# A three-layer kernel on one core: batch 1's first spectrum chunk comes second, and the weight splits follow the first tile's reads

## The chip, the core and the metric

The kernel runs on one core of a Trainium2 chip. The core has five engines with an instruction stream each: TensorE (PE: matmuls; PEld: its weight loads), VectorE (DVE), ScalarE (ACT), GpSimd (POOL) and SyncE (SP, which here only issues DMAs). They are synchronised by semaphores. Sixteen DMA engines serve the core. The metric is the device time of one launch in microseconds, the median of several runs.

## The reference

Three layers on x of 2 batches x 3008 positions x 256 channels, all in float32:

```python
X = np.fft.rfft(x, axis=1)                 # layer 1: a filter in the spectrum
y = np.fft.irfft(X * (filt_r + 1j * filt_i)[None], n=3008, axis=1)

x = y.reshape(6016, 256)                   # layer 2: normalised, gated
xn = x / np.sqrt(np.mean(x * x, -1, keepdims=True) + 1e-6) * rms_g
g = xn @ w_gate                            # 256 x 1536
x = (silu(g) * (xn @ w_val)) @ w_out       # 1536 x 256

r = np.maximum(x @ w_in, 0)                # layer 3: 256 x 2048
out = (s * (r * r) + b) @ w_out2           # 2048 x 256
```

The filter is the same for both batches.

## The kernel before, in words

**Spectrum stage.** 3008 = 47 x 64, and the transform is done by tables in four matmul steps. The 256 channels of a batch are cut into 8 chunks, so there are 16 chunks, `q` = 0 to 15, taken in the order of their numbers: first all of batch 0, then all of batch 1. For chunk q: `load_x(q)` brings 384 KB into one of three slots (it waits until step 1 of chunk q-3 has read the slot); TensorE's `step1` (8 matmuls) transforms along 47; ScalarE's `u_out` copies the result out of PSUM; `step2` transforms along 64. VectorE's `products(q, dp)`, dp = 0 and 1, multiplies by the filter with three instructions each; GpSimd's `total(q, dp)` adds the two parts into `spec`; TensorE's `step3(q, dp)` starts the way back and ScalarE's `w_out_copy(q, dp)` puts it into `w_fft` of its batch. `store_w` writes half a batch (four chunks) of that to `by_j` in DRAM, and `load_z` reads it back in another arrangement for `step4`, which finishes the transform for one tile of 376 tokens. There are 16 such tiles.

A filter chunk is 768 KB. There are 8, one for each chunk of a batch. `load_f(n)` loads it, and GpSimd's `sign(n)` then multiplies its imaginary part by signs from the table, before VectorE may use it. Filters stay in SBUF, so that batch 1's chunks (q = 8 to 15) need no load.

TensorE's order in the loop for q from 3: `step2(q)`, `step3(q-1, 0)`, `step1(q+1)` in two halves, `step3(q-1, 1)`. Step 4 of token tiles 0 and 1 is placed into the iterations q = 10, 12, 14 and 15. GpSimd's order is `total(q, 0)`, `total(q, 1)`, then the signing of the filter for a later chunk, or weight splits, or the squares of a token tile.

**Layers 2 and 3.** Each float32 operand is split into a high part (rounded) and a low part (the rest), and `split_product` makes one product of three matmuls. Weights are split on the way: ScalarE makes the high part (`w1_high`, `w1d_high`), and GpSimd (`w1_low`, for the gate and value weights) or VectorE (`w1d_low`, for the down weights) subtracts it from the raw weights. The gate and value weights come in 16 pieces, two for each entry of `ORDER1` = (0, 0), (0, 1), (1, 0), (0, 2), (1, 1), (0, 3), (1, 2), (1, 3), where the first number is 0 for gate and 1 for value and the second is the block of 384 columns. So pieces 0 to 5 hold gate blocks 0 and 1 and value block 0, pieces 6 and 7 gate block 2, pieces 8 and 9 value block 1.

For token tile t and block c of 128 hidden columns (c = 0 to 11), TensorE does `gate_val(t, par, c)`, 12 matmuls, called product c in the prediction, and two blocks later `down(t, par, c)`, 6 matmuls, called down product c. In tile 0, product 0 waits for 6 split pieces, product 3 for 10, product 6 for 14 and product 9 for 16. Between them ScalarE makes the silu, VectorE the product `h` (`hmul`), ScalarE its high part and VectorE its low part (`low`). Down product 0 waits for `low(0, 0)` and for the first down split `w1d_low(0)`. `squares`, `square_sum` and `square_split` on GpSimd prepare the normalisation of a tile, and TensorE's `sums` adds it up.

**What sets the order.** Everything is written out by hand: an engine takes its instructions in the order of the code and stops at the first one whose semaphore isn't there. All DMAs are issued by SyncE, so a DMA behind a waiting one waits too.

Of the kernel before, what the change touches and what calls it, by code (L numbers as in the profile page):

```python
# [21 lines left out]
P = 128  # L22
# [11 lines left out]
PAIRS = 8  # L34
# [12 lines left out]
PIECES1 = 4 * BLOCKS1  # L47
PIECES1D = 2 * BLOCKS1
ORDER1 = ((0, 0), (0, 1), (1, 0), (0, 2), (1, 1), (0, 3), (1, 2), (1, 3))
PIECE2O = 512  # L50
# [46 lines left out]
def build(nc, by_j, x, filt, tab, small, w_gate, w_val, w_out, w_in2, w_out2, out):  # L97
    with ExitStack() as ctx:
# [139 lines left out]
        def _(sp):  # L238
# [6 lines left out]
            def load_f(n):  # L245
                sp.dma_start(f_tiles[n][:].rearrange("p k c -> p (k c)"), filt[n]).then_inc(f_in[n], 16)

            def store_w(b, half):

                sp.wait_ge(w_done, CHUNKS * (2 * b + half + 1))  # L250
                sp.dma_start(by_j[b, half].rearrange("p j d -> p (j d)"),
                             w_fft[b][:, half].rearrange("p j d -> p (j d)")).then_inc(w_stored[b][half], 16)
# [11 lines left out]
            sp.dma_start(tabs[:, 0:TB2], tab[:, 0:TB2]).then_inc(tab1_in, 16)  # L264
            load_x(1)
            load_f(0)
            sp.dma_start(tabs[:, TB2:], tab[:, TB2:]).then_inc(tab2_in, 16)
            load_x(2)
            load_f(1)
            load_f(2)  # L270
            for q in range(3, 8):
                load_x(q)
                load_f(q)
            load_x(8)
            load_x(9)
            store_w(0, 0)
            load_x(10)
            sp.dma_start(consts[:], small).then_inc(consts_in, 16)
            load_x(11)
            sp.wait_ge(w_stored[0][0], 16)  # L280
            for t in range(2):
                load_z(0, 0, t * GROUPS * XROWS, t)
            load_gate(0)
            store_w(0, 1)
            load_x(12)
            load_x(13)
# [244 lines left out]
        def _(a):  # L531
# [7 lines left out]
            def w_out_copy(q, dp):  # L539
                b, n = q // CHUNKS, q % CHUNKS  # L540
                a.wait_ge(s3_mm, 2 * q + dp + 1)
                n, d0 = n * HALVES // CHUNKS, (2 * n + dp) * PAIRS * HALVES % P
                nc.scalar.copy(w_fft[b][:, n, :, d0:d0 + PAIRS * HALVES],
                               bank[6][:, 0:COLS].rearrange("p (d j) -> p j d", j=NJ)).then_inc(w_done, 1)
# [206 lines left out]
        def _(dve):  # L751
            nc.vector.memset(warm[:], 1.0).then_inc(warm_set, 1)
            def products(q, dp):

                dve.wait_ge(s2_mm, q + 1)
                if q < CHUNKS:
                    dve.wait_ge(f_signed, q + 1)
                if q:
                    dve.wait_ge(spec_done, 2 * (q - 1) + dp + 1)
                xs = bank[2 + 2 * (q % 2) + dp]  # L760
                f = f_tiles[q % CHUNKS]
                cols = slice(dp * COLS, (dp + 1) * COLS)
# [57 lines left out]
            hmul(0, 0)  # L820
            hmul(0, 1)
            low(0, 0)
            w1d_low(0)

# [74 lines left out]
        def _(gp):  # L899
# [44 lines left out]
            gp.wait_ge(tab1_in, 16)  # L944
            for n in range(2):
                sign(n)
            for q in range(ALL):
                total(q, 0)
                total(q, 1)
                if q + 2 < CHUNKS:  # L950
                    sign(q + 2)
                elif q == 11:
                    for i in range(3):
                        w1_low(i)
                elif q == 12:
                    squares(0)
                    square_sum(0)
                    square_split(0)
                elif q == 13:
                    for i in range(3, 6):  # L960
                        w1_low(i)
                elif q == 15:
                    w1_low(6)
                    w1_low(7)

            def body(t, par, last):
# [4 lines left out]
                if is0(t):  # L971
                    for i in range(8, PIECES1):
                        w1_low(i)
                    gp.wait_ge(in2_in, 16)
# [53 lines left out]
```

## Time and profile before

| | us |
|---|---|
| median of 3 runs (lowest, highest) | 1257.45 (1256.34, 1257.88) |
| profiled execution, its own time | 1262.11 |
| its span, first to last instruction | 1260.3 |
| TensorE busy in it | 1245.2 |
| VectorE, ScalarE, GpSimd busy | 679.3, 554.1, 161.9 |

The spectrum stage takes about the first 100 us, layers 2 and 3 the rest. The mean granted TensorE clock is 0.995 of full speed. A timeline row gives start, duration, engine, line, operation, output and inputs, and how often; in brackets stands for how long the engine was idle before it and what released it. Rows of neighbouring instructions of a kind are merged. The trace counts a float32 matmul of the spectrum stage twice, so that one step 2 of a chunk, 4 matmuls, is a row of x8. "Old time axis" below means the times of this profiled execution.

### The profile page before, as it was taken

How to read it: one execution, taken by the hardware profiler on the slowest of the kernel's cores; microseconds unless marked ns; L12 is line 12 of the kernel's file. 1: busy time of each engine (PE TensorE's matmuls, PEld its weight loads, DVE VectorE, ACT ScalarE, POOL GpSimd, SP SyncE). 2: the span in 40 equal slices, each digit the busy share in tenths (PEclk: the TensorE clock that was granted, in tenths of full speed). 3: DMA queues.
4: the chain of work that ended last, by engine and by line, in shares of the span. 5: the costliest groups of instructions: out<-in, count | busy, mean ns of one | idle time of the engine just before them, and what ended most of it. 6: DMA issues, size and time to landing. Idle time of an engine off the chain costs nothing.

```text
span 1260.3 us, 20452 instructions
## 1 busy us (share of the span) xinstructions
PE 1245.2 (99%) x7268; PEld 1214.0 (96%) x7268; DVE 679.3 (54%) x1141; ACT 554.1 (44%) x1111; POOL 161.9 (13%) x167
## 2 busy tenths in 40 slices
PE   8998999999999999999999999999999999999998
PEld 5677999999999999999999999999999999999998
DVE  4675455444454444544454375555555555555555
ACT  2365333333434334343344364555454545554554
POOL 5665111011110111101120030000000000000000
PEclk9998999999999999999999999999999999999999
DMA  9863000000000000000010000000000000000000
GB/s 236 272 217 154 14 13 14 1 13 12 13 12 1 11 12 12 12 3 10 0 67 1 1 1 14 13 13 12 12 12 12 12 12 12 12 12 12 13 6 20
DMA packets 22519, 41.07 MB, mean 33 GB/s; under 512 B 1872, under 2 KB 18384, under 8 KB 21456
## 3 DMA queue, kind: packets, MB, share of 16 engines
q1 hardware_dynamic: 22480, 40.55, 10.4%
q8 instruction: 24, 0.39, 0.1%
q14 instruction: 15, 0.12, 0.0%
HBM read 28.10 MB, written 12.45 MB: 32 GB/s over the span
## 4 chain that ended last, share of the span: by engine, by line
PE 91%; POOL 4%; issue 3%; DMA 1%; SPq 0%; DVE 0%; POOLq 0%
PE bank L388 30%; PE bank L389 30%; PE bank L390 30%; POOL spec L916 2%; PE bank L373 2%; DMA f<-filt 1%; POOL gate_lo L921 0%; POOL val_lo L921 0%; POOL sq L931 0%; PE bank L385 0%; PE bank L384 0%; POOL f L909 0%; POOL sq L935 0%; SPq L243 0%; POOL ss_lo L942 0%
## 5 line engine op out<-in xcount | busy, mean ns | idle before, releaser
L801 DVE TENSOR_TENSOR h<-bank,act 128x376 f32<-128x376 f32 x192 | 104.5, 545 | 314.8 <-PE bank L390 307.7
L832 DVE SCALAR_TENSOR_TENSOR h<-act,consts 128x376 f32<-128x376 f32 x256 | 159.6, 623 | 189.5 <-ACT act L667 185.5
L573 ACT ACTIVATE act<-bank 128x376 f32<-128x376 f32 x192 | 92.9, 484 | 363.3 <-PE bank L390 363.0
L667 ACT ACTIVATE act<-bank 128x376 f32<-128x376 f32 x256 | 124.0, 484 | 224.0 <-PE bank L390 223.9
L390 PE MATMUL bank<-h_hi,out_lo 128*128 128x376 f32 x512 | 171.4, 335 | 0.0
L389 PE MATMUL bank<-h_lo,out_hi 128*128 128x376 f32 x512 | 171.4, 335 | 0.0
L388 PE MATMUL bank<-xn_hi,in_hi 128*128 128x376 f32 x512 | 171.2, 334 | 0.2 <-issue 0.2
L388 PE MATMUL bank<-h_hi,out_hi 128*128 128x376 f32 x512 | 171.2, 334 | 0.0
L389 PE MATMUL bank<-xn_lo,in_hi 128*128 128x376 f32 x512 | 171.1, 334 | 0.0
L390 PE MATMUL bank<-xn_hi,in_lo 128*128 128x376 f32 x512 | 170.3, 333 | 0.0
L838 DVE SCALAR_TENSOR_TENSOR h_lo<-h,consts,h_hi 128x376 fp32r<-128x376 f32 x256 | 157.7, 616 | 0.2 <-ACT h_hi L676 0.2
L676 ACT ACTIVATE h_hi<-h,consts 128x376 fp32r<-128x376 f32 x256 | 154.2, 603 | 1.9 <-DVE h L832 1.9
L388 PE MATMUL bank<-xn_hi,gate_hi 128*128 128x376 f32 x384 | 131.6, 343 | 2.8 <-POOL val_lo L921 2.7
L388 PE MATMUL bank<-h_hi,down_hi 128*128 128x376 f32 x384 | 128.7, 335 | 1.7 <-DVE down_lo L775 1.7
L389 PE MATMUL bank<-xn_lo,val_hi 128*128 128x376 f32 x384 | 129.3, 337 | 0.0
L390 PE MATMUL bank<-h_hi,down_lo 128*128 128x376 f32 x384 | 128.9, 336 | 0.0
L389 PE MATMUL bank<-h_lo,down_hi 128*128 128x376 f32 x384 | 128.8, 335 | 0.0
L388 PE MATMUL bank<-xn_hi,val_hi 128*128 128x376 f32 x384 | 128.7, 335 | 0.0
L389 PE MATMUL bank<-xn_lo,gate_hi 128*128 128x376 f32 x384 | 128.6, 335 | 0.0
L390 PE MATMUL bank<-xn_hi,val_lo 128*128 128x376 f32 x384 | 128.6, 335 | 0.0
L390 PE MATMUL bank<-xn_hi,gate_lo 128*128 128x376 f32 x384 | 128.5, 335 | 0.0
L809 DVE TENSOR_TENSOR h_lo<-h,h_hi 128x376 fp32r<-128x376 f32 x192 | 118.4, 617 | 1.4 <-ACT h_hi L582 1.3
(79 smaller groups left out, 2041.3 us busy)
## 6 DMA issues: line engine op xcount, KB each, us to landing
x_ring<-x SPq DMA_DIRECT2D x16, 384.0 KB, 7.5
f<-filt SPq DMA_DIRECT2D x8, 768.0 KB, 15.0
by_j<-w_b SPq DMA_DIRECT2D x4, 1536.0 KB, 6.1
z_ring<-by_j SPq DMA_DIRECT2D x32, 192.0 KB, 2.8
out<-staged SPq DMA_DIRECT2D x32, 188.0 KB, 1.9
in_raw<-w_in SPq DMA_DIRECT2D x1, 2048.0 KB, 8.7
out_raw<-w_out SPq DMA_DIRECT2D x1, 2048.0 KB, 7.7
gate_raw<-w_gate SPq DMA_DIRECT2D x2, 768.0 KB, 7.2
```

What stands on the lines that cost most here:

```text
L373: mm = nc.tensor.matmul(bank[7][:, k * BM:(k + 1) * BM], z_ring[:, par, half, k], s4m, start=True, stop=True)
L388: nc.tensor.matmul(acc, hi, xh, start=first, stop=False)
L389: nc.tensor.matmul(acc, hi, xl, start=False, stop=False)
L390: return nc.tensor.matmul(acc, lo, xh, start=False, stop=final)
L573: nc.scalar.activation(act[:, c % 2], bank[2 * (c % 2)][:, 0:TILE], ACT.Silu).then_inc(silu_done, 1)
L667: nc.scalar.activation(act[:, c % 2], bank[c % 4][:, 0:TILE], ACT.Relu).then_inc(relu_done, 1)
L676: nc.scalar.activation(h_hi[:, c % 4], h[:, c % 2], ACT.Identity, bias=bi2).then_inc(gh_done, 1)
L801: nc.vector.tensor_tensor(h[:, c % 2], bank[2 * (c % 2) + 1][:, 0:TILE], act[:, c % 2], ALU.mult).then_inc(hmul_done, 1)
L809: nc.vector.tensor_tensor(h_lo[:, c % 4], h[:, c % 2], h_hi[:, c % 4].bitcast(F32), ALU.subtract).then_inc(hl_done, 1)
L832: nc.vector.scalar_tensor_tensor(out=h[:, c % 2], in0=act[:, c % 2], scalar=sc2, in1=act[:, c % 2], op0=ALU.mult, op1=ALU.mult).then_inc(q ...
L838: nc.vector.scalar_tensor_tensor(out=h_lo[:, c % 4], in0=h[:, c % 2], scalar=bi2, in1=h_hi[:, c % 4].bitcast(F32), op0=ALU.add, op1=ALU.su ...
L916: nc.gpsimd.tensor_tensor(spec[:, q % 2, dp], prod[:, dp, 0], prod[:, dp, 1], ALU.add).then_inc(spec_done, 1)
```

## The change

1. The 16 chunks are taken in the order `ORDER`: batch 0 chunk 0, batch 1 chunk 0, then batch 0 chunks 1 to 7, then batch 1 chunks 1 to 7. `q` now counts places in this order. Place 0 and place 1 both use filter 0, and place q up to 8 uses filter q-1. The host arranges x in that order. `products`, `w_out_copy` and `store_w` look up their chunk in `ORDER`; so the stores of batch 0's halves wait for 10 and 18 copies, where 8 and 16 were waited for.
2. SyncE issues the second table before filter 0, and filter q-1 behind x chunk q. `load_x(12)` stands ahead of the first wait for a store.
3. GpSimd signs one filter before its loop, and then filter q+1 behind the sums of chunk q.
4. GpSimd's splits of the gate and value weights stand in other places: two pieces after chunk 11 (three before), four after chunk 13 (three), two after chunk 14 (none), two after chunk 15 (two, but now pieces 8 and 9).
5. VectorE does `w1d_low(0)` before `low(0, 0)`.

```diff
+ORDER = [(0, 0), (1, 0)] + [(0, n) for n in range(1, CHUNKS)] + [(1, n) for n in range(1, CHUNKS)]
...
-                sp.wait_ge(w_done, CHUNKS * (2 * b + half + 1))
+                sp.wait_ge(w_done, 2 * ORDER.index((b, CHUNKS // HALVES * (half + 1) - 1)) + 2)
...
             load_x(1)
+            sp.dma_start(tabs[:, TB2:], tab[:, TB2:]).then_inc(tab2_in, 16)
             load_f(0)
-            sp.dma_start(tabs[:, TB2:], tab[:, TB2:]).then_inc(tab2_in, 16)
-            load_x(2)
-            load_f(1)
-            load_f(2)
-            for q in range(3, 8):
+            for q in range(2, 9):
                 load_x(q)
-                load_f(q)
-            load_x(8)
+                load_f(q - 1)
             load_x(9)
             store_w(0, 0)
             load_x(10)
             sp.dma_start(consts[:], small).then_inc(consts_in, 16)
             load_x(11)
+            load_x(12)
             sp.wait_ge(w_stored[0][0], 16)
...
             store_w(0, 1)
-            load_x(12)
             load_x(13)
...
             def w_out_copy(q, dp):
-                b, n = q // CHUNKS, q % CHUNKS
+                b, n = ORDER[q]
...
             def products(q, dp):
                 dve.wait_ge(s2_mm, q + 1)
-                if q < CHUNKS:
-                    dve.wait_ge(f_signed, q + 1)
+                dve.wait_ge(f_signed, ORDER[q][1] + 1)
...
-                f = f_tiles[q % CHUNKS]
+                f = f_tiles[ORDER[q][1]]
...
             hmul(0, 1)
+            w1d_low(0)
             low(0, 0)
-            w1d_low(0)
...
-            for n in range(2):
-                sign(n)
+            sign(0)
             for q in range(ALL):
                 total(q, 0)
                 total(q, 1)
-                if q + 2 < CHUNKS:
-                    sign(q + 2)
+                if q + 1 < CHUNKS:
+                    sign(q + 1)
                 elif q == 11:
-                    for i in range(3):
+                    for i in range(2):
                         w1_low(i)
...
                 elif q == 13:
-                    for i in range(3, 6):
+                    for i in range(2, 6):
                         w1_low(i)
-                elif q == 15:
-                    w1_low(6)
-                    w1_low(7)
+                elif q >= 14:
+                    w1_low(2 * (q - 11))
+                    w1_low(2 * (q - 11) + 1)
...
-                    for i in range(8, PIECES1):
+                    for i in range(10, PIECES1):
                         w1_low(i)
```

On SyncE at the program's start (`f_50` is filter 0, `f_51` filter 1 and so on; `tabs` of 128x384 is the second table), before:

```order
L243 DMA x_ring<-x 96x1024
L264 DMA tabs<-tab 128x120
L243 DMA x_ring<-x 96x1024
L246 DMA f_50<-filt 128x1536
L267 DMA tabs<-tab 128x384
L243 DMA x_ring<-x 96x1024
L246 DMA f_51<-filt 128x1536
L246 DMA f_52<-filt 128x1536
L243 DMA x_ring<-x 96x1024
L246 DMA f_53<-filt 128x1536
```

and now:

```order
L244 DMA x_ring<-x 96x1024
L265 DMA tabs<-tab 128x120
L244 DMA x_ring<-x 96x1024
L267 DMA tabs<-tab 128x384
L247 DMA f_50<-filt 128x1536
L244 DMA x_ring<-x 96x1024
L247 DMA f_51<-filt 128x1536
L244 DMA x_ring<-x 96x1024
L247 DMA f_52<-filt 128x1536
L244 DMA x_ring<-x 96x1024
L247 DMA f_53<-filt 128x1536
```

The second table has moved ahead of filter 0, and there is an x chunk between any two filters.

On GpSimd from the sums of chunk 13 (`spec`) to the splits behind the squares of token tile 1 (`sq`, `ss_hi`, `ss_lo`), before:

```order
L916 TENSOR_TENSOR spec<-prod 128x384 x2
L921 TENSOR_TENSOR gate_lo<-gate_raw,gate_hi 128x384
L921 TENSOR_TENSOR val_lo<-val_raw,val_hi 128x384 x2
L916 TENSOR_TENSOR spec<-prod 128x384 x4
L921 TENSOR_TENSOR gate_lo<-gate_raw,gate_hi 128x384 x2
L931 TENSOR_TENSOR sq<-y 128x752
L935 TENSOR_TENSOR sq<-sq 128x376
L940 CAST ss_hi<-sq 128x376
L942 TENSOR_TENSOR ss_lo<-sq,ss_hi 128x376
L921 TENSOR_TENSOR val_lo<-val_raw,val_hi 128x384 x2
```

and now:

```order
L912 TENSOR_TENSOR spec<-prod 128x384 x2
L917 TENSOR_TENSOR gate_lo<-gate_raw,gate_hi 128x384 x2
L917 TENSOR_TENSOR val_lo<-val_raw,val_hi 128x384 x2
L912 TENSOR_TENSOR spec<-prod 128x384 x2
L917 TENSOR_TENSOR gate_lo<-gate_raw,gate_hi 128x384 x2
L912 TENSOR_TENSOR spec<-prod 128x384 x2
L917 TENSOR_TENSOR val_lo<-val_raw,val_hi 128x384 x2
L927 TENSOR_TENSOR sq<-y 128x752
L931 TENSOR_TENSOR sq<-sq 128x376
L936 CAST ss_hi<-sq 128x376
L938 TENSOR_TENSOR ss_lo<-sq,ss_hi 128x376
```

Pieces 6 and 7 (`gate_lo`) have moved between the sums of chunks 14 and 15, and pieces 8 and 9 (`val_lo`) from behind the squares of tile 1 to ahead of them.

On VectorE right behind the last products, with the first blocks of token tile 0, before:

```order
L801 TENSOR_TENSOR h<-bank,act 128x376 x2
L809 TENSOR_TENSOR h_lo<-h,h_hi 128x376
L775 TENSOR_TENSOR down_lo<-down_raw,down_hi 128x384
L801 TENSOR_TENSOR h<-bank,act 128x376
L809 TENSOR_TENSOR h_lo<-h,h_hi 128x376
L775 TENSOR_TENSOR down_lo<-down_raw,down_hi 128x384
```

and now:

```order
L797 TENSOR_TENSOR h<-bank,act 128x376 x2
L771 TENSOR_TENSOR down_lo<-down_raw,down_hi 128x384
L805 TENSOR_TENSOR h_lo<-h,h_hi 128x376
L797 TENSOR_TENSOR h<-bank,act 128x376
L805 TENSOR_TENSOR h_lo<-h,h_hi 128x376
L771 TENSOR_TENSOR down_lo<-down_raw,down_hi 128x384
```

The first down split and the low part of the first h have changed places.

## Rows read from the trace of the kernel before

**Rows 1.** Of the page, part 1: busy time, share of span, instructions.

```profile
PE 1245.2 (99%) x7268; PEld 1214.0 (96%) x7268; DVE 679.3 (54%) x1141; ACT 554.1 (44%) x1111; POOL 161.9 (13%) x167
```

**Rows 2.** View of waits, TensorE, whole span: us in total, times, longest.

```profile
PE bank L388 <- POOL val_lo L921: 2.7, 1, 2.7
...
PE bank L362 <- POOL spec L916: 2.4, 4, 0.9
PE bank L388 <- DVE down_lo L775: 1.7, 1, 1.7
```

**Rows 3.** Windows: busy us of each engine, granted clock, DMA share, GB/s.

```profile
20.00:45.00 25.00, 23.51 (x139) 15.41 (x136) 17.27 (x32) 9.09 (x19) 18.12 (x15) 1.00 1.02 240
13.40:16.30 2.90, 2.90 (x12) 1.28 (x8) 2.02 (x4) 0.00 (x0) 1.01 (x1) 0.50 1.08 338
105.60:112.20 6.60, 6.11 (x19) 6.11 (x20) 1.89 (x3) 2.11 (x5) 4.41 (x5) 0.50 0.78 268
```

**Rows 4.** Timeline, GpSimd, start: start us, us, instruction, idle before and releaser.

```profile
10.96 1.80 POOL L909 TENSOR_TENSOR f<-f,tabs 128x768 f32<-128x768 f32 x1 [6.95 <-DMA f<-filt]
...
21.31 1.95 POOL L916 TENSOR_TENSOR spec<-prod 128x384 f32<-128x384 f32 x2
...
45.37 1.81 POOL L909 TENSOR_TENSOR f<-f,tabs 128x768 f32<-128x768 f32 x1 [2.11 <-DMA f<-filt]
```

**Rows 5.** Timeline, TensorE, spectrum stage.

```profile
12.22 4.48 PE L352 MATMUL bank<-u_ring,tabs 64*128 64x384 f32 x16 [2.47 <-DMA tabs<-tab]
...
23.11 1.92 PE L341 MATMUL bank<-tabs,x_ring 128*128 128x96 f32 x16
...
25.63 1.56 PE L352 MATMUL bank<-u_ring,tabs 64*128 64x384 f32 x8
...
51.46 1.56 PE L352 MATMUL bank<-u_ring,tabs 64*128 64x384 f32 x8
...
56.22 1.56 PE L352 MATMUL bank<-u_ring,tabs 64*128 64x384 f32 x8
...
72.90 1.13 PE L373 MATMUL bank<-consts,z_ring 96*128 96x94 f32 x8
```

**Rows 6.** Timeline, VectorE, first and last product of chunk 0.

```profile
14.19 0.56 DVE L763 TENSOR_TENSOR prod<-bank,f 128x384 f32<-128x384 f32 x1 [12.78 <-PE bank L352]
...
17.13 0.55 DVE L765 TENSOR_TENSOR prod<-bank,f 64x384 f32<-64x384 f32 x1
```

**Rows 7.** Timeline, SyncE's queue, batch 0's second store and its z loads.

```profile
56.84 0.37 SPq L251 DMA_DIRECT2D by_j<-w_b  x1
...
63.12 0.85 SPq L255 DMA_DIRECT2D z_ring<-by_j  x2
```

**Rows 8.** Of the page, part 6: count, KB each, us from issue to landing.

```profile
z_ring<-by_j SPq DMA_DIRECT2D x32, 192.0 KB, 2.8
```

**Rows 9.** Timeline, GpSimd, first token tile.

```profile
97.16 2.00 POOL L921 TENSOR_TENSOR gate_lo<-gate_raw,gate_hi 128x384 fp32r<-128x384 f32 x2
...
104.10 1.93 POOL L921 TENSOR_TENSOR val_lo<-val_raw,val_hi 128x384 fp32r<-128x384 f32 x2
```

**Rows 10.** Timeline, VectorE, first token tile.

```profile
98.47 1.09 DVE L809 TENSOR_TENSOR h_lo<-h,h_hi 128x376 fp32r<-128x376 f32 x1 [1.30 <-ACT h_hi L582]
99.49 1.79 DVE L775 TENSOR_TENSOR down_lo<-down_raw,down_hi 128x384 fp32r<-128x384 f32 x1
```

**Rows 11.** Timeline, TensorE, first token tile.

```profile
101.42 0.41 PE L388 MATMUL bank<-h_hi,down_hi 128*128 128x376 f32 x1 [1.68 <-DVE down_lo L775]
101.67 0.34 PE L389 MATMUL bank<-h_lo,down_hi 128*128 128x376 f32 x1
...
102.53 0.81 PE L362 MATMUL bank<-spec,tabs 128*128 128x384 f32 x2
106.09 0.68 PE L388 MATMUL bank<-xn_hi,gate_hi 128*128 128x376 f32 x1 [2.75 <-POOL val_lo L921]
...
111.90 0.51 PE L388 MATMUL bank<-xn_hi,gate_hi 128*128 128x376 f32 x1
```

## What the change was predicted to do

> **What bounds the kernel now.** I read the page first. It gives TensorE as busy for 99% of the span [rows 1], so the only things that can change the time are the stretches in which TensorE waits and those in which it works at the lower of its two clock levels. The view of waits then says where TensorE stands still: 2.7 us once for the GpSimd split of the value weights, 2.4 us over four waits for the GpSimd sum of the spectrum, 1.7 us once for the VectorE split of the down weights [rows 2]. With the 2.47 us of wait for the second table [rows 5] nearly all lies before 110 us; the remaining 1,150 us is matmul behind matmul, which the change doesn't touch. So I read the first 112 us only, by windows and by timeline, engine by engine.
>
> The windows show two things [rows 3]. From 20 to 45 us the DMA engines are busy for their whole time (share 1.02, 240 GB/s): the spectrum stage is paced by transfers there. And there are two stretches at granted clock 0.50, which is 1.2 GHz, from about 13.4 to 16.3 us and from 105.6 to 112.2 us. Each came with or right after an idle gap of TensorE, of 2.47 us and of 2.75 us with 1.68 us shortly before it [rows 5, 11].
>
> GpSimd shows how the transfers pace the stage [rows 4]: it waits for filter n to land, signs it in 1.8 us, and only then makes the sum that lets the chunk before go on. The last filter lands at 45.37 us. TensorE's iteration 3 (counted by the chunk of its step 2) starts at 25.63 us and iteration 8 at 51.46 us; from 8 to 9 it takes 4.76 us, with TensorE without a gap [rows 5]. Five iterations at that pace are 23.8 us, and they took 25.83 us: about 2.0 us is lost to filters there, and the rest of the loss lies ahead of iteration 3.
>
> **Part 1, one filter fewer in front of every chunk.** Chunk q now needs filter q-1. Ahead of chunk q's filter stand 768 KB less, which at the 240 GB/s of the window is 3.3 us. That is the ceiling of this part if transfers alone decide. What decides first is the start, so I walk it.
>
> The second table now follows the second x chunk and has no filter in front. It must land by about 9.7 us, where TensorE ends step 1 of both chunks (12.22 less 2.47 idle). Only 192 KB, under 1 us, come after an x chunk that has been used by then, so I take this wait of 2.47 us as gone. Filter 0 takes the place that the table had: the same bytes have passed, so I let it land when the table did, at 12.22 us [rows 5]; it may be 0.4 us earlier, since filter 0 alone came at 10.96 us and only 192 KB are added. From there: sign 1.80 us [rows 4], to 14.02. The six products of chunk 0 take 3.49 us (14.19 to 17.68, [rows 6]), to 17.54. The second sum is 0.98 us (half of a pair of 1.95 to 1.96), to 18.5. Then GpSimd signs filter 1 (1.8 us; it has landed by then, since no byte more stands in front of it than before, and chunk 1's sum, which comes after its signing and three products of 1.7 us, began at 21.31, so that it lay there by 17.8), to 20.3, and makes the first sum of chunk 1, to 21.3. Before, that sum ended at 22.29 us (start 21.31), and iteration 3 began 3.34 us later. So iteration 3 now starts at about 24.65 us, 1.0 us earlier.
>
> Iterations 3 to 7 then need filters 2 to 6 in the place of 3 to 7, and TensorE's own pace of 4.76 us puts iteration 8 at 48.45 us, 3.0 us earlier. Filter 7 is the check: the bytes up to it are those of before plus one x chunk (384 KB, 1.6 us), so it lands at about 47.0 us; sign, sum and hand-over (2.8 us) give 49.8 us, and step 3 that needs it comes 1.5 us into iteration 8, at 49.95. That is hardly a margin. I take **2.8 us** for this part, with 1.8 us (filter 7 a microsecond late) and 3.3 us (the bytes' ceiling) as its ends.
>
> From iteration 8 on, what comes earlier must not run into loads that don't. The store of batch 0's second half waits for a chunk later than before (18 copies for 16): issued at 56.84 us before, now 4.76 us later by place and 2.8 us earlier by pace, 58.8 us. The z loads behind it could go 6.3 us after the store (56.84 to 63.12, [rows 7]), so now at 65.1, and land 2.8 us after their issue [rows 8], by 68.3 with the second issue. TensorE's step 4 for them stood at 72.90 us [rows 5] and stands at 70.1 now. Clear by 1.8 us. The x chunk that moved ahead of the first z loads, and the gate weights behind those, have more room by the same working, so these edits cost 0.
>
> **Part 2, weight splits in the order of reading.** TensorE's gate and value product number 3 waits for pieces 8 and 9. GpSimd made them at 104.10 us, behind the squares and sums of token tile 1, which nobody needed then [rows 9]. It now makes pieces 6 and 7 ahead of chunk 15's sums and 8 and 9 behind them. Pieces 6 and 7 ended at 99.16 (97.16 plus 2.00); the same work in another order ends there at the latest, and since the timeline has GpSimd idle between the sums of chunks 14 and 15 for most of the two pieces' time, I take 97.6. Pieces 8 and 9 are then done at about 99.6 us on the old time axis, 101.1 at the latest. TensorE comes to product 3 at 102.1 (1.92 us after down product 0 starts, as 103.34 stands to 101.42, [rows 11]; part 3 has that start). ScalarE has their high halves by then: it makes them ahead of the second silu, whose product VectorE had finished at 97.17 us (98.47 less 1.30 idle, [rows 10]). Chunk 15's sums are over by 97.6, and their first matmul stood at 98.9 (101.42 less 1.68 idle less its own 0.8). So the wait of 2.75 us goes. What is queued behind, the squares, takes its 5 us (99.16 to 104.10) from 99.6 and is done at 104.7; TensorE's sums of tile 1 come after product 5, at about 111.
>
> **Part 3, the two VectorE instructions exchanged.** Before, VectorE stood idle for 1.30 us for the high part of h, then made the low part (1.09 us), then the down split (1.79 us), and TensorE's down product began at 101.42 us after 1.68 us of waiting [rows 10, 11]. Now the split runs in that idle time: 97.17 plus 1.79 is 98.96, plus 1.09 is 100.05, and TensorE starts at about 100.15. The wait shrinks to 0.4 us. Its ends: 1.68 (the exchange brings nothing) and 0 (the split is fast). Both instructions read two operands in SBUF, and they took 1.79 us beside a busy GpSimd. The Trainium skill, in "GPSIMD Engine Reference", Key points, says that GpSimd shares its SBUF interfaces with VectorE, with contention for instructions of two SBUF inputs. The trace fits it with the 1.79 us, and the rule speaks against any hope of a fast split here, since the change puts more GpSimd work ahead of 97 us and not less.
>
> **Part 4, the clock.** With 4.43 us of idle time shrunk to 0.4, the second low stretch has no gap in front of it. Products 3 with their down product, 18 matmuls from 106.09 to 111.90 us, took 5.81 us [rows 11]; five matmuls between 101.67 and 102.53 us stood 0.172 us apart, so 18 take 3.10. That is 2.7 us, and 0.2 us for the three matmuls after 111.90 that ran partly slow. Parts 2 to 4 together: 2.75 + 1.68 - 0.4 + 2.9 = **6.9 us**; ends 5.6 (the exchange brings nothing) and 7.3.
>
> Sum: 2.8 + 6.9 = 9.7 us. The profiled execution took 1262.1 us, so it would take 1252.4; the median of the runs shown is 4.7 us lower, and I take the same difference off it: 1257.45 - 9.7 = **1247.8 us**. Its own range, with the ends of both terms, is 1246.8 to 1250.1.
>
> **Rivals.** First, **the clock falls at the start again.** The change removes one gap but makes two: TensorE ends step 2 of two chunks at 12.9 us (9.75 and twice 1.56), has 1.9 us of step 1 for chunk 2 [rows 5], and stands until chunk 0's first sum at about 17 (half the products and 0.98 us after 14.02), 2.2 us in all; then it waits about 1.5 us more, to 21.3, for the sum behind the signing. Before, 2.47 us in one piece was enough [rows 3, 5]. Against it: work lies between these pieces. A low stretch of 3 us there doubles about 1.5 us of work: gain 8.2 us, 1249.3. At the length of the second one (6.6 us) it costs 3.3: 1251.1. A sentence apart: the Trainium skill, "TensorE: Matmul & The Clock Gate", Part 1, says that how many matmuls run slow at a kernel's start varies from run to run; by that rule this rival would come in some runs and not in others.
>
> Second, **the start's gain doesn't last**: filter 7, or a transfer further back, is late by as much as the loop gained, and TensorE meets chunk 15 no earlier. For it speaks that the margins above are 0.1 to 1.8 us; against it, that the bytes are fewer. Gain 6.9, 1250.6 us.
>
> Third, **the split wait comes back one step later.** Product 6 needs pieces 12 and 13, which GpSimd now makes after squares and pieces 10 and 11, at about 108.7 us, and TensorE arrives at 111.7. A GpSimd slowed by VectorE could lose those 3 us and more. Gain 4 to 5.6 us in all, 1252.6.
>
> Fourth, **slower**: the z loads. SP issues in order, and step 4 of tile 0 is in TensorE's fixed order. If the store, now a chunk later, and the loads queued behind it slip by more than 1.8 us, TensorE waits in iteration 12, each us costs one, the clock may fall on top (3 us), and everything behind on SP (x chunks, value weights) slips too. It decides the sign from a slip of 1.8 + 9.7 - 3 = 8.5 us; at 12 us the time is about 1261. The DMA engines were far from full there, so I give it little.
>
> **Chances.** Forecast 0.62, clock at the start 0.15, start's gain lost 0.08, split wait returns 0.06, no change for a reason that I don't see 0.05, slower 0.04. 0.2% is 2.5 us, about what a measurement can tell; all of the first four are past it, so faster 0.91, same 0.05, slower 0.04. The range goes up to 1252.0, which takes in the first three cases and part of the fourth, and down to 1245.8: both terms at their high ends (10.6 us) are 1246.8, and a microsecond for the spread of the runs.
>
> **What would show it.** The wait for the second table gone and filter 0 landing near 12.2 us; iteration 3 near 24.7 and iteration 8 near 48.5 us, with no longer wait there than 0.3 us; step 4 of tile 0 without a wait; the value split ending near 97 us on the new axis; down product 0 waiting under 0.6 us, product 3 not at all, and a granted clock of 1.00 from the start's end on. I am wrong if a clock of 0.50 shows between 17 and 30 us, if iteration 8 starts after 49.7, or if a new wait on GpSimd stands at product 6.

## The result, and the profile after

| | before | after |
|---|---|---|
| median of 4 runs each (lowest, highest), us | 1257.66 (1256.34, 1259.76) | 1249.22 (1248.59, 1250.03) |
| profiled execution, its own time | 1262.11 | 1250.03 |
| its span | 1260.3 | 1248.2 |

The ratio is 0.9932, with a 95% interval of 0.9914 to 0.9949: 8.6 us faster (6.4 to 10.8), and 1249.2 us measured against 1247.8 forecast. The two profiled executions differ by 12.1 us and the medians by 8.4; where the rest comes from turned out to be the interesting part.

Of the page after, part 1, which answers to [rows 1]:

```profile
PE 1239.7 (99%) x7268; PEld 1210.3 (97%) x7268; DVE 680.4 (55%) x1141; ACT 554.1 (44%) x1111; POOL 164.1 (13%) x167
```

TensorE's waits in the kernel after, over the whole span (us in total, times, longest), which answer to [rows 2]:

```profile
PE bank L359 <- POOL spec L912: 2.6, 2, 1.4
PE bank L330 <- DVE warm L749: 1.5, 1, 1.5
PE bank L381 <- POOL ss_lo L938: 0.6, 1, 0.6
PE bank L338 <- DMA x_ring<-x: 0.3, 1, 0.3
```

The waits for the value split, the down split and the second table are gone. The 1.5 us for `warm` lie at the program's very start, before the first matmul, and were the same in the kernel before. What is left otherwise of more than 0.6 us is the wait for GpSimd's sum, twice, before the first `step3` of chunks 0 and 1: the two gaps that the prediction's first rival had.

Windows of the kernel after (busy time of each engine, granted clock, DMA share, GB/s). The first holds the first of those gaps, the others answer to [rows 3]:

```profile
12.00:16.00 4.00, 2.51 (x18) 2.16 (x18) 3.18 (x6) 0.96 (x2) 1.55 (x2) 1.00 1.04 257
20.00:45.00 25.00, 25.00 (x147) 16.67 (x147) 17.70 (x32) 9.78 (x21) 20.94 (x17) 1.00 1.02 277
95.00:112.00 17.00, 17.00 (x97) 16.50 (x96) 13.63 (x16) 11.50 (x23) 12.94 (x13) 1.00 0.57 217
```

The clock is 1.00 in all of them. From 20 to 45 us TensorE is busy for all of its time, and the DMA engines still are too, at 277 GB/s where the profiled execution of before had 240.

TensorE's timeline after (start, duration, instruction, in brackets the idle time before it), with the rows that answer to [rows 5, 11]. In order they are step 2 of the first two chunks in one row, the first step 3 of chunks 0 and 1, iterations 3 and 8, step 4 of tile 0, down product 0, and products 3 and 4:

```profile
8.95 2.85 PE L349 MATMUL bank<-u_ring,tabs 64*128 64x384 f32 x16
...
15.52 0.91 PE L359 MATMUL bank<-spec,tabs 128*128 128x384 f32 x2 [1.40 <-POOL spec L912]
...
20.00 0.91 PE L359 MATMUL bank<-spec,tabs 128*128 128x384 f32 x2 [1.24 <-POOL spec L912]
...
23.28 1.56 PE L349 MATMUL bank<-u_ring,tabs 64*128 64x384 f32 x8
...
47.10 1.56 PE L349 MATMUL bank<-u_ring,tabs 64*128 64x384 f32 x8
...
68.55 1.13 PE L370 MATMUL bank<-consts,z_ring 96*128 96x94 f32 x8
...
94.82 0.59 PE L385 MATMUL bank<-h_hi,down_hi 128*128 128x376 f32 x1
...
96.46 0.62 PE L385 MATMUL bank<-xn_hi,gate_hi 128*128 128x376 f32 x1
...
99.97 0.34 PE L385 MATMUL bank<-xn_hi,gate_hi 128*128 128x376 f32 x1
```

Iteration 8 starts at 47.10 us instead of 51.46. Down product 0 and product 3 follow without any gap, and product 4, which began at 111.90 us, begins at 99.97.

GpSimd and VectorE after, which answer to [rows 4, 9, 10]: filter 0 and filter 1 signed; the splits of pieces 6 and 7 and of 8 and 9; the down split ahead of the low part of h:

```profile
10.75 1.81 POOL L905 TENSOR_TENSOR f<-f,tabs 128x768 f32<-128x768 f32 x1 [6.74 <-DMA f<-filt]
...
17.19 1.81 POOL L905 TENSOR_TENSOR f<-f,tabs 128x768 f32<-128x768 f32 x1
...
89.15 1.98 POOL L917 TENSOR_TENSOR gate_lo<-gate_raw,gate_hi 128x384 fp32r<-128x384 f32 x2
...
93.02 2.60 POOL L917 TENSOR_TENSOR val_lo<-val_raw,val_hi 128x384 fp32r<-128x384 f32 x2
95.59 1.43 POOL L927 TENSOR_TENSOR sq<-y 128x752 f32<-128x752 f32 x1
```

```profile
92.58 0.90 DVE L771 TENSOR_TENSOR down_lo<-down_raw,down_hi 128x384 fp32r<-128x384 f32 x1
94.13 0.63 DVE L805 TENSOR_TENSOR h_lo<-h,h_hi 128x376 fp32r<-128x376 f32 x1 [0.65 <-ACT h_hi L579]
```

Pieces 8 and 9 are done at 95.62 us, 0.8 us before product 3 would read them, and the squares of tile 1 start behind them.

### The profile page after: what moved, and what is told of

It reads as the page before. It is cut to its first block, busy times and chain, and to the rows that moved or that the text cites. A ratio compares the mean times of both kernels' runs of the same rounds, so it can differ in the third digit from the quotient of the medians.

```text
span 1248.2 us, 20452 instructions
## 1 busy us (share of the span) xinstructions
PE 1239.7 (99%) x7268; PEld 1210.3 (97%) x7268; DVE 680.4 (55%) x1141; ACT 554.1 (44%) x1111; POOL 164.1 (13%) x167
## 4 chain that ended last, share of the span: by engine, by line
PE 95%; POOL 2%; issue 1%; DMA 1%; DVE 1%; SPq 0%; POOLq 0%; DVEq 0%
PE bank L385 30%; PE bank L386 30%; PE bank L387 30%; PE bank L370 2%; POOL spec L912 1%; PE bank L359 1%; PE bank L349 1%; PE bank L338 1%; DMA f<-filt 1%; POOL f L905 0%; PE bank L381 0%; PE bank L382 0%; DVE prod L761 0%; DVE prod L760 0%; POOL gate_lo L917 0%
```

## The experiments

All were timed in turns with the kernel before on the same chip. In each, "us under before" is the ratio applied to 1256.5 us.

**The kernel before once more.**

> The kernel before once more, with its own profile. Theory A (the clock theory): the profiled execution of before (1262.1 us) was 4.6 us over the median of its runs because its two stretches at granted clock 0.50 aren't the same in every execution; then the executions here spread over some 3 to 6 us, the mean granted clock goes with the time (a longer execution shows a lower clock), and this profile shows low stretches of another length or place. Rival B: a profiled execution is simply 4.6 us longer; then this one takes about 1262 again with the same two low stretches, and all others 1257 to 1258 at one clock.

Measured: 1256.53 us in 12 runs and 1256.53 in 29 of the kernel before beside them (ratio 0.9997, 0.9986 to 1.0007). The profiled execution took 1256.44 us with a mean clock of 1.000. TensorE's waits and timeline in it:

```profile
PE bank L388 <- POOL val_lo L921: 2.8, 1, 2.8
PE bank L362 <- POOL spec L916: 1.8, 1, 1.8
PE bank L352 <- DMA tabs<-tab: 1.7, 1, 1.7
PE bank L388 <- DVE down_lo L775: 1.7, 1, 1.7
```

```profile
17.54 0.91 PE L362 MATMUL bank<-spec,tabs 128*128 128x384 f32 x2 [1.81 <-POOL spec L916]
...
24.69 1.56 PE L352 MATMUL bank<-u_ring,tabs 64*128 64x384 f32 x8
...
48.52 1.56 PE L352 MATMUL bank<-u_ring,tabs 64*128 64x384 f32 x8
...
103.17 0.44 PE L388 MATMUL bank<-xn_hi,gate_hi 128*128 128x376 f32 x1 [2.75 <-POOL val_lo L921]
...
106.39 0.34 PE L388 MATMUL bank<-xn_hi,gate_hi 128*128 128x376 f32 x1
```

The two waits in front of the first tile's products stand to a tenth of a microsecond as in [rows 2], but the clock never falls: products 3 and their down product take 3.22 us (103.17 to 106.39) where they took 5.81 in [rows 11]. And the stage isn't paced by filters: from iteration 3 to 8 it takes 23.83 us, which is TensorE's own pace, against 25.83 in [rows 5]. So theory A holds, and more than it said: the one trace on which my sum rested was the slow end in two ways. Over all 73 executions of the kernel before in these experiments, 22 have a mean granted clock of 1.000, with a median of 1255.2 us, and 51 have 0.999 or less, with 1257.1. None of the 73 took as long as the profiled 1262.11.

**The chunk order alone.**

```diff
 (of the kernel after)
-            w1d_low(0)
             low(0, 0)
+            w1d_low(0)
...
-                    for i in range(2):
+                    for i in range(3):
                         w1_low(i)
...
```

The second edit, with three more of its kind behind it, puts GpSimd's splits back where the kernel before has them.

> Only the new order of chunks, filters, tables and signs; GpSimd's splits and VectorE's two instructions as before. Traces of before and after say that iteration 8 starts 4.4 us earlier (51.46 to 47.10), so by theory A the time falls by 4.4 us less what of the start's low clock an average execution didn't have: 3 to 4.4 us, and the waits for the value split (2.7 us) and the down split (1.7 us) stand as before. Rival B: by my prediction's sum it is 2.8 us. A third, that the parts aren't additive: the end loses what the start gains, under 1.5 us.

Measured: 1255.16 us, ratio 0.9982 (0.9973 to 0.9992): 2.3 us under before (1.0 to 3.4). TensorE's waits and iterations 3 and 8:

```profile
PE bank L385 <- POOL val_lo L917: 2.7, 1, 2.7
...
PE bank L385 <- DVE down_lo L771: 1.7, 1, 1.7
```

```profile
22.07 1.56 PE L349 MATMUL bank<-u_ring,tabs 64*128 64x384 f32 x8
...
45.89 1.56 PE L349 MATMUL bank<-u_ring,tabs 64*128 64x384 f32 x8
```

Both end waits are where they were, and in this trace the clock did fall behind them (0.50 from 102 to 104 us). The interval holds the prediction's 2.8 us, and theory A's 3 to 4.4 only at its edge.

**The splits and the exchange alone.**

```diff
 (of the kernel before)
+            w1d_low(0)
             low(0, 0)
-            w1d_low(0)
...
-                elif q == 15:
-                    w1_low(6)
-                    w1_low(7)
+                elif q >= 14:
+                    w1_low(2 * (q - 11))
+                    w1_low(2 * (q - 11) + 1)
...
```

The numbers of pieces after chunks 11 and 13 are those of the change too (two and four), and tile 1's loop begins with piece 10.

> Only GpSimd's splits at their new places and VectorE's exchange, chunks in the old order. Both waits in token tile 0 should be gone: 4.4 us, and where an execution had the low clock behind them up to 2.9 us more. Theory A, with low clock in only part of the executions of before: 4.4 to 6 us in the median, and a profile with granted clock 1.00 from 20 us on. Rival B (low stretch in every execution of before): 6.9 to 7.7 us.

Measured: 1250.03 us, ratio 0.9943 (0.9927 to 0.9958), 7.2 us under before (5.3 to 9.2). A second time, beside the changed kernel on one chip:

> Splits and exchange alone, chunks in the old order, beside the changed kernel. Theory A: 1 to 1.5 us over the changed kernel. Rival B: the same time, so the last 2.3 us that the chunk order won alone (with the old splits) came from somewhere that the new splits win too, such as the clock.

> The changed kernel, on one chip with the splits and exchange alone. Theory A, the chunk order brings 1.5 us more on top of them (from the traces: iteration 8 starts 36.4 us after filter 0 lands in the new order, 37.9 or more in the old, and filter 0 lands up to 0.8 us later): about 1 to 1.5 us under the other. Rival B, nothing on top: within 0.5 us of it.

Measured: 1250.60 us, ratio 0.9954 (0.9940 to 0.9968), 5.8 us under before (4.0 to 7.5), and the changed kernel 1249.06 us, ratio 0.9942 (0.9928 to 0.9955). For the splits and the exchange the first timing lies with rival B (6.9 to 7.7) and the second with theory A (4.4 to 6); each interval reaches into both, so these times alone don't decide between them.

The chunk order on top brings 1.5 us here, as theory A had it. Each of the five runs of the changed kernel is under each of the other's five, while the ratios' intervals overlap; with all runs of the two kernels together the difference is 1.2 (1250.53 in 11 runs, 1249.29 in 14). So the size is less sure than the sign. The second trace of the splits alone shows something else that the chunk order changes. Filter 0 lands at 9.27 us in it, and TensorE's timeline has:

```profile
16.30 1.49 PE L362 MATMUL bank<-spec,tabs 128*128 128x384 f32 x2 [1.43 <-POOL spec L916]
17.73 2.62 PE L352 MATMUL bank<-u_ring,tabs 64*128 64x384 f32 x8
...
48.92 1.56 PE L352 MATMUL bank<-u_ring,tabs 64*128 64x384 f32 x8
```

The clock falls behind the gap at chunk 0's step 3 (the window from 16 to 18 us has 0.63), and iteration 8 starts 39.65 us after filter 0 landed. In the first trace of this kernel the clock stays at 1.00 and it is 37.92 (8.30 to 46.22 us).

**The changed kernel beside others.**

> The changed kernel once more, beside the others. The two parts measured alone were 2.3 us (chunk order) and 7.2 us (splits and exchange). Theory A, the parts add up: 9.4 us under before, with every mean granted clock at 1.0 because no gap in front of the first token tile is left. Rival B, the parts overlap: what the chunk order wins in an average execution is mostly gone once the splits are in place; then about 8 us or less, as the first timing said (8.4).

Measured: 1249.51 us, ratio 0.9941 (0.9929 to 0.9954), 7.4 us under before (5.8 to 8.9). 2.3 plus 7.2 is 9.5, over the interval, while with the second timing of the splits (5.8 us) the parts add to 8.1. I can't tell from these whether they overlap. In 13 of the changed kernel's 14 executions the mean clock is 1.000 (the other, the profiled one here with 0.999, has no low stretch before 1240 us); in the kernel before it was so in 22 of 73.

**The gaps filled, the waits left.**

```diff
+            def fill(n):
+                for _ in range(n):
+                    nc.tensor.matmul(bank[7][:, 0:TILE], ones_r[:], xn_hi[:, 0, 0], start=True, stop=True)
...
+                    if is0(t) and c == 1:
+                        pe.wait_ge(y_done, 4)
+                        fill(14)
...
+                        fill(8)
                     down(t, par, c)
```

The 8 stand ahead of down product 0, the 14 ahead of product 3, both in tile 0 alone.

> The kernel before with 8 extra matmuls in front of down product 0 and 14 in front of product 3 of token tile 0, whose results aren't used; they fill the two waits (1.4 of 1.7 us, 2.4 of 2.7 us) and leave what is waited for as it is. It measures the clock alone. Theory A: TensorE still starts product 3 at about 106 us, but at granted clock 1.00, so the median falls by the share of executions that had the low stretch times 2.9 us: 1 to 2.9 us. If the low clock doesn't come from the gaps: 0 or a little slower (up to 0.6 us).

Measured: 1255.32 us, ratio 0.9986 (0.9977 to 0.9995): 1.8 us under before (0.6 to 2.9). 9 of 12 executions have a mean clock of 1.000. The timeline of TensorE shows the extra matmuls and what they leave:

```profile
96.65 1.84 PE L482 MATMUL bank<-xn_hi,ones_r 128*128 128x376 f32 x8
98.80 0.41 PE L388 MATMUL bank<-h_hi,down_hi 128*128 128x376 f32 x1 [0.30 <-DVE down_lo L784]
...
100.25 2.88 PE L482 MATMUL bank<-xn_hi,ones_r 128*128 128x376 f32 x14
103.51 0.44 PE L388 MATMUL bank<-xn_hi,gate_hi 128*128 128x376 f32 x1 [0.38 <-POOL val_lo L930]
...
106.73 0.34 PE L388 MATMUL bank<-xn_hi,gate_hi 128*128 128x376 f32 x1
```

Product 3 still waits for its weights, now 0.38 us, and TensorE gets nothing done earlier; what is won is the clock alone. So 22 useless matmuls make the kernel faster, as theory A had it, and the clock's share of the loss at the end is about 1.8 us in an average execution, where my sum had 2.9 in every one. The interval just reaches that 2.9.

**The exchange undone.**

```diff
 (of the kernel after)
-            w1d_low(0)
             low(0, 0)
+            w1d_low(0)
```

> The changed kernel with VectorE's two instructions back in their old order. By my sum the exchange is worth 1.3 us (a wait of 1.7 us at down product 0 shrinks to 0.4; the trace of the changed kernel even shows 0). Theory A: 1.3 to 1.7 us over the changed kernel, with a wait of 1.3 to 1.7 us at down product 0, granted clock still 1.00, since the other gap behind it is gone. Rival B: the freed GpSimd order makes the old order harmless, under 0.3 us of wait.

Measured: 1251.80 us, ratio 0.9960 (0.9947 to 0.9973), 2.3 us over the changed kernel on the same chip (1249.51), each of its five runs over each of the other's. VectorE and TensorE, and a window of the clock:

```profile
92.89 1.31 DVE L805 TENSOR_TENSOR h_lo<-h,h_hi 128x376 fp32r<-128x376 f32 x1 [1.46 <-ACT h_hi L579]
94.12 1.79 DVE L771 TENSOR_TENSOR down_lo<-down_raw,down_hi 128x384 fp32r<-128x384 f32 x1
```

```profile
96.06 0.55 PE L385 MATMUL bank<-h_hi,down_hi 128*128 128x376 f32 x1 [2.05 <-DVE down_lo L771]
```

```profile
96.50:99.50 3.00, 3.00 (x9) 2.39 (x8) 1.43 (x2) 0.01 (x1) 2.79 (x4) 0.50 0.00 0
```

The wait is 2.05 us, longer than the old 1.68, since the low part takes 1.31 us and not 1.09, with GpSimd at the value splits beside it, and starts after 1.46 us of idle time and not 1.30. And this one gap was enough: the clock stands at 0.50 behind it, and in 2 of 5 executions the mean is 0.998. I had the clock at 1.00 in this kernel; that expectation failed. The three executions at 1.000 have a median of 1251.25 us, 1.7 over the changed kernel, and the two at 0.998 took 1252.42 and 1252.58, about 3 over it. So the exchange is worth its wait and, in some executions, the clock on top.

**The table alone.**

```diff
+            sp.dma_start(tabs[:, TB2:], tab[:, TB2:]).then_inc(tab2_in, 16)
             load_f(0)
-            sp.dma_start(tabs[:, TB2:], tab[:, TB2:]).then_inc(tab2_in, 16)
```

> The kernel before with the second table's load ahead of filter 0 and nothing else. Theory A: the wait of 1.7 to 2.5 us for the table goes from TensorE, but the signed filters set the pace right behind it: 0 to 0.7 us in time, and longer waits of TensorE for GpSimd's sum take the place. Rival B: the wait was worth its length, about 2 us, and then the chunk order itself brought nothing.

Measured: 1257.56 us, ratio 1.0009 (1.0000 to 1.0019): no gain, rather 1.1 us slower (0 to 2.4), where theory A had 0 to 0.7 us of gain. TensorE's timeline and a window:

```profile
8.87 2.85 PE L352 MATMUL bank<-u_ring,tabs 64*128 64x384 f32 x16
...
15.42 1.44 PE L362 MATMUL bank<-spec,tabs 128*128 128x384 f32 x2 [1.74 <-POOL spec L916]
16.79 2.68 PE L352 MATMUL bank<-u_ring,tabs 64*128 64x384 f32 x8
```

```profile
16.00:18.60 2.60, 2.60 (x8) 1.18 (x8) 2.44 (x6) 0.48 (x1) 2.60 (x3) 0.50 1.01 323
```

TensorE starts step 2 at 8.87 us with no wait, and gets nothing from it, because chunk 0's sum isn't there before. The wait has moved from in front of step 2 to in front of step 3, and behind it the clock falls: the step 2 that takes 1.56 us elsewhere takes 2.68. 11 of 12 executions are below a mean clock of 1.000, against 51 of 73 of the kernel before. This is the first rival of the prediction, in the old chunk order.

**Less to transfer.**

```diff
-                sp.dma_start(x_ring[0:XROWS, q % XRING].rearrange("p i c -> p (i c)"), x[q]).then_inc(x_in[q % XRING], 16)
+                rows = XROWS if q < XRING else 16
+                sp.dma_start(x_ring[0:rows, q % XRING].rearrange("p i c -> p (i c)"), x[q][0:rows]).then_inc(x_in[q % XRING], 16)
```

> The kernel before, but from chunk 3 on only 16 of the 96 rows of x are loaded (the others are those of an earlier chunk): 320 KB less per chunk for the transfers, everything else the same. It takes the pacing by transfers out of the spectrum stage and leaves the rest. Theory A: the filters' lateness that I read in the one trace of before (2 us between iterations 3 and 8) is the exception, the other traces of the old start have 0 to 0.7 us: gain 0.3 to 1 us. Rival B, as my prediction had it: transfers pace the stage in every execution: gain 2 us or more.

Measured: 1256.40 us against 1256.42, ratio 0.9999 (0.9990 to 1.0008). The kernel leaves out 80 of the 96 rows of x from chunk 3 on, so its results are of no use and only its time is. Taking these 320 of the 1152 KB (x and filter) that belong to a chunk away moves nothing that can be measured. One of its windows:

```profile
25.00:45.00 20.00, 20.00 (x117) 12.98 (x117) 13.33 (x24) 8.35 (x18) 14.55 (x12) 1.00 0.47 171
```

From 25 to 45 us the DMA engines are busy for 0.47 of their time here, and TensorE is busy for all of it, at the pace that it has in the other traces with the full load. The interval goes from 1.3 us faster to 1.0 slower: it rules out rival B's 2 us, and leaves theory A's 0.3 to 1 us open. (In this trace, too, the clock falls at the start, behind a gap of 1.59 us: 0.50 from 18 to 20 us.)

**Further on at the start.**

```diff
 (of the kernel after; TensorE, with ScalarE's copies in the same order)
             step3(0, 1)
-            step3(1, 0)
             step1(3, 0)
             step1(3, 1)
+            step3(1, 0)
             step3(1, 1)
...
                 total(q, 0)
+                if q == 0:
+                    sign(1)
+                if q == 12:
+                    squares(0)
                 total(q, 1)
...
```

> The changed kernel with three places moved on: filter 1 is signed between the two sums of chunk 0 (0.7 us off the sum of chunk 1), TensorE does step 1 of chunk 3 ahead of the first step 3 of chunk 1 (fills the wait of 1.2 us), and GpSimd squares tile 0 between the two sums of chunk 12 (0.6 us wait at sums). Theory A: the trace shows iteration 3 about 1.5 us earlier, and no wait at the sums: 1.5 to 2.0 us under the changed kernel, with the same 4.76 us a chunk. Rival B: filters then arrive too late at that pace, a wait for a filter comes back in iterations 4 to 8 and half or more of it is lost: under 0.8 us.

Measured: 1248.04 us, ratio 0.9933 (0.9920 to 0.9946), 1.5 us under the changed kernel on the same chip (1249.51), the intervals overlapping. Its waits:

```profile
PE bank L359 <- POOL spec L912: 1.2, 2, 0.9
PE bank L359 <- ACT w_b L540: 0.7, 1, 0.7
```

```profile
22.71 1.56 PE L349 MATMUL bank<-u_ring,tabs 64*128 64x384 f32 x8
...
46.53 1.56 PE L349 MATMUL bank<-u_ring,tabs 64*128 64x384 f32 x8
```

The wait at the sums is gone (0.6 us). At the start less was won than the 1.5 us that I expected: iteration 8 starts 36.15 us after filter 0 lands (10.38 us), and 36.35 in the kernel after (10.75 us). A wait of 0.7 us on ScalarE has come in. GpSimd waits for no filter after the first, so rival B's reason doesn't hold either. It has the lowest median of all kernels here.

## Why the prediction came out right, and where it was off

**The splits.** Right in place and about right in size. Product 3 no longer waits, and no wait came back at product 6, whose pieces were done at 104.98 us, 1.5 us ahead of it. From iteration 8 to product 4, TensorE takes 57.87 us in the second trace of before (48.52 to 106.39, clock at 1.00 all the way) and 52.87 after (47.10 to 99.97). The other traces at that clock agree: 57.85 to 57.91 with the old waits (the table alone, less to transfer, the gaps filled), 52.86 to 52.89 with the new splits (the changed kernel twice more, the splits alone twice). So the two waits are worth 5.0 us without any clock; my sum had 4.0 (4.43 less 0.4). The 0.4 was the down product's rest of a wait, which is 0. I had held a fast split to be out of hope, since GpSimd would be busy then, and that step was wrong in its size: the down split took 0.90 us in its new place and not 1.79, while GpSimd ended chunk 15's sums beside it and had only just begun to split. That the company makes the difference is read from these rows, not tested. The rest, 0.6 us, I put to the refill of TensorE behind two gaps, also untested.

**The clock.** The step "2.7 us, and 0.2 us" took the low stretch of one execution for one of all. It is there in part of the executions: of the five traces with both old waits open, the clock fell behind them in two, where iteration 8 to product 4 took 60.44 us (the first of before) and 59.38 (the order alone), 2.6 and 1.5 us more than the 57.87 without. Filling the gaps without removing the waits gave 1.8 us (0.6 to 2.9). Parts 2 to 4 were forecast at 6.9 us and measured alone at 7.2 and 5.8. The two errors, 1.0 us too little for the waits and about 1 us too much for the clock, went against each other, so it was luck in part that 6.9 is so near.

**The chunk order.** Forecast 2.8, measured 2.3 alone and about 1.2 to 1.5 on top of the rest. Its places all came earlier than forecast: filter 0 landed at 10.75 us for 12.2, iteration 3 started at 23.28 for 24.65 and iteration 8 at 47.10 for 48.45. The five iterations between took 23.82 us, as worked out; what was off was where the chain at the start begins.

Here the size was near and one reason was wrong. "Transfers pace the stage", which I read off a DMA share of 1.02 and 2.0 us of filter waits, isn't so in every execution. Of the seven traces of the old order, two show a wait for a late filter between iterations 3 and 8: the first of before with 2.0 us, and the one with the gaps filled with 1.0:

```profile
45.55 0.91 PE L362 MATMUL bank<-spec,tabs 128*128 128x384 f32 x2 [1.03 <-POOL spec L925]
```

In an average execution, 320 of 1152 KB less per chunk change nothing that can be measured.

What the order does change is the chain at the start. In the old order GpSimd signs filter 1 ahead of chunk 0's sums, and filter 1 lands some 4 us after filter 0 (10.96 and 15.29 us in the first trace of before), so TensorE stands for 1.81 us in front of chunk 0's step 3 in the second trace of before. In the new order the sums don't wait for it. Iteration 8 starts 36.4 us after filter 0 lands in the new order (10.75 to 47.10 after, 9.53 to 45.89 with the order alone, and 36.4 to 36.5 in three more traces) and 38.0 in the old one without filter waits and without a low clock (10.49 to 48.52, and 37.92 in the first trace of the splits alone). That is 1.6 us, less what filter 0 loses by the table ahead of it. That filter 1's place is the cause of all of the 1.6 is argued from these rows; I moved it alone in no run, and the old order also has a wait of 0.66 us for ScalarE ahead of iteration 3 (at 21.45 us in the second trace of before) that the kernel after doesn't have.

On top comes the clock at the start. It is low in four of the seven traces of the old order and in none of the six of the new one, and where it is low behind chunk 0's step 3, iteration 8 starts up to 1.7 us later still (39.65 and 39.75 us after filter 0 in the second trace of the splits alone and in that with less to transfer). The prediction had this only as a risk of the new order. How much of the 1.2 to 2.3 us is this clock, the runs don't tell.

How early filter 0 lands varies from execution to execution by over 2 us (8.30 to 10.96 us in the six traces with the loads in the old order), which no working from one trace could see. The 4.4 us between the first two traces at iteration 8 are the 1.6, the 2.0 us of filter waits of one execution, and 0.8 that are left over; I put these to its low clock and its later filter 0.

**The table.** The prediction counted 2.47 us of wait as gone and then found by the chain at the start that only 1.0 of it counts at iteration 3. That caution was right: the table alone brings nothing, since what is removed from one place of TensorE is waited for in the next.

**The rivals.** The clock falling at the start was the wrong way round for this kernel: it falls there in the old order (in the first trace of before, with the table first, in the second trace of the splits alone, and in that with less to transfer), and in none of the three traces of the kernel after. Why is open: their gap in front of chunk 0's step 3 is 1.40, 0.36 and 0.57 us, and the second, in front of chunk 1's, 1.23 or 1.24. The start's gain did last, since iterations 3 to 8 have no gap.

The z loads had room: step 4 of tile 0 at 68.55 us has no wait. But the reason that I gave, that the DMA engines were far from full there, was a misreading. A window of the kernel before over the store and these loads shows them nearly full:

```profile
57.00:65.00 8.00, 8.00 (x53) 5.58 (x49) 5.61 (x11) 2.59 (x6) 3.22 (x4) 1.00 0.95 309
```

So this fourth rival deserved more weight than that reason left it.

**The reference.** My sum of 9.7 us was taken off the median, though its durations came from an execution 4.7 us over it. The measured difference of 8.4 (7.4 and 7.3 when measured again) is between that and nothing: some of the sum consisted of what made that execution long.

## What to carry to other kernels

Before a sum is made of one profiled execution, its own time is to be set beside the other runs: where it is longer, look for what is in it and may not be in the others, which here were a low clock behind gaps and late transfers, and count these by their share. A gap of TensorE costs its length and, in some of the executions, a low clock behind it, here 1.5 to 2.6 us more; so order the side work of GpSimd and VectorE by what TensorE reads next, and try the two instructions that swap for free. A wait that is removed at the head of a chain is worth something only if the next thing in the chain is ready; a busy DMA share isn't by itself a bound (TensorE worked all of the 25 us from 20 to 45 at a share of 1.02 in the kernel after).

## What the hardware showed that I had not expected

Twenty-two matmuls whose results nobody reads made the kernel 1.8 us faster (0.6 to 2.9), by keeping the granted clock up. A single gap of 2.05 us, with 17 us of unbroken work right ahead of it, let the clock fall to 0.50 for about 3 us in one trace (the exchange undone), while gaps of 1.68 and 2.75 us with 1.9 us of work between let it fall in one trace of the kernel before and not in the other. At the start it fell behind gaps of 1.43, 1.59 and 1.74 us in front of chunk 0's step 3 (the second trace of the splits alone, less to transfer, the table alone), and not behind one of 1.81 us in the second trace of before: the length of a gap alone doesn't tell. The same first filter of 768 KB landed between 8.30 and 10.96 us in six traces of one order of loads.
